# Attention scores made two query tiles at a time, with the q_high by k_low products in the two row halves of the array

## What is computed

```python
def _attn_ref(q, k, v, w1, b1, w2):          # q, k, v: (4, 8, 576, 64)
    scores = scale * np.matmul(q, k.transpose(0, 1, 3, 2))
    ...                                       # bias of each head from the relative position
    scores = scores + bias.transpose(2, 0, 1)[None, :, :, :]
    scores = scores - np.max(scores, axis=-1, keepdims=True)
    attn = np.exp(scores)
    attn = attn / (np.sum(attn, axis=-1, keepdims=True) + 1e-09)
    return np.matmul(attn, v)
def _moe_ref(x, w_in, w_out):
    h = x @ w_in
    return (h * np.cos(h)) @ w_out
def _moe2_ref(x, w_gate, w_val, w_out, rms_g):
    ...                                       # RMS norm, then silu(xn @ w_gate) * (xn @ w_val) @ w_out
```

## Time and profile before

| what | value |
|---|---|
| device time, median of 3 runs | 1208.93 us (1208.05 to 1209.38) |
| device time of the profiled execution | 1208.74 us |
| its span, first to last instruction | 1207.0 us |
| mean granted clock of the tensor engine | 0.996 of full speed |
| PE busy over the span | 97% |
| DVE, ACT, POOL busy over the span | 58%, 41%, 41% |
| first and last score matmul | 68.0 us and 325.2 us |

### The profile page before, as it was taken

One profiled execution on the slowest core, in us unless ns is written; L12 is line 12 of the kernel. 1 busy time (PEld: TensorE's weight loads), 2 busy tenths in 40 slices (PEclk: granted clock), 3 DMA queues, 4 the chain that ended last, 5 costly groups with the idle time before them and its releaser, 6 DMA issues. The chain is left out here.

```text
span 1207.0 us, 21829 instructions
## 1 busy us (share of the span) xinstructions
PE 1171.1 (97%) x7464; PEld 1078.6 (89%) x7464; DVE 704.4 (58%) x1540; ACT 496.3 (41%) x1034; POOL 490.4 (41%) x515
## 2 busy tenths in 40 slices
PE   5789999999989999999999999999999999999998
PEld 2267777777779999999999999999999999999998
DVE  8978888888889867777786887553011020210201
ACT  6967787787723433333343333111111111111111
POOL 3047777777766342525243362751111111111111
PEclk9989999999999999999999999999999999999999
DMA  5754535252144000000000011330000000000000
GB/s 172 247 174 126 170 99 170 100 188 81 56 114 123 18 2 1 0 0 0 0 0 0 0 36 35 105 114 27 1 1 26 0 26 0 0 26 0 26 0 26
DMA packets 46534, 69.06 MB, mean 57 GB/s; under 512 B 3712, under 2 KB 27424, under 8 KB 46496
## 3 DMA queue, kind: packets, MB, share of 16 engines
q1 hardware_dynamic: 46496, 68.60, 18.3%
HBM read 53.25 MB, written 15.34 MB: 57 GB/s over the span
## 5 line engine op out<-in xcount | busy, mean ns | idle before, releaser
L820 PE MATMUL banks<-x_high,w_low_rest 128*128 128x384 f32 x672 | 224.5, 334 | 0.0
L818 PE MATMUL banks<-x_high,w_high_rest 128*128 128x384 f32 x672 | 224.4, 334 | 0.0
L819 PE MATMUL banks<-x_low,w_high_rest 128*128 128x384 f32 x672 | 224.4, 334 | 0.0
L1367 DVE TENSOR_TENSOR X<-X,banks 128x384 f32<-128x384 f32 x72 | 39.8, 552 | 298.6 <-PE banks L820 298.5
L1386 POOL TENSOR_TENSOR product_low<-X,product_high 128x384 fp32r<-128x384 f32 x72 | 72.8, 1012 | 345.5 <-ACT product_high L1329 345.5
L1184 POOL TENSOR_TENSOR product_low<-g,product_high 128x384 fp32r<-128x384 f32 x96 | 102.3, 1066 | 236.9 <-ACT product_high L1066 236.9
L818 PE MATMUL bank<-product_high,w_high_rest 128*128 128x384 f32 x480 | 162.1, 338 | 0.8 <-POOL product_low L1184 0.8
L820 PE MATMUL bank<-product_high,w_low_rest 128*128 128x384 f32 x480 | 160.5, 334 | 0.0
L819 PE MATMUL bank<-product_low,w_high_rest 128*128 128x384 f32 x480 | 160.5, 334 | 0.0
L1094 ACT ACTIVATE angle<-angle,quarter 128x384 f32<-128x384 f32 x96 | 59.3, 617 | 201.9 <-DVE angle L1126 201.9
L644 DVE CUSTOM_DVE_ANT_0 probs<-banks,bias 128x576 f32<-128x576 f32 (+1 forms) x160 | 119.7, 748 | 20.6 <-PE banks L506 10.0
(11 more groups left out here) (113 smaller groups left out, 2525.4 us busy)
## 6 DMA issues: line engine op xcount, KB each, us to landing
raw_qk<-in_qk SPq DMA_DIRECT2D x32, 576.0 KB, 3.8
bias_scratch<-bias_stage SPq DMA_DIRECT2D x36, 288.0 KB, 3.2
bias<-bias_scratch SPq DMA_DIRECT2D x32, 288.0 KB, 3.4
w_raw<-in_w_out SPq DMA_DIRECT2D x28, 256.0 KB, 2.7
values<-in_v SPq DMA_DIRECT2D x16, 320.0 KB, 4.1
w_raw<-in_w_in SPq DMA_DIRECT2D x16, 256.0 KB, 2.9
out_t<-X SPq DMA_DIRECT2D x5, 768.0 KB, 3.6
w_raw<-in_w_gate SPq DMA_DIRECT2D x12, 256.0 KB, 3.3
```

The costliest lines, as they stand in the source:

```text
L818: nc.tensor.matmul(out, high, x_high, start=start, stop=False)
L819: nc.tensor.matmul(out, high, x_low, start=False, stop=False)
L820: return nc.tensor.matmul(out, low, x_high, start=False, stop=stop)
```

## The change

Tiles are scored in twos, s and s+1 with s even. Of each tile the two matmuls with `k_high` stay as they are (128 rows of the array; `both_parts`). The two with `k_low` now use the 64 partitions that hold q_high, and the other 64, q_low by k_low, are not computed any more. So that the two tiles of a two use different halves of the array, q_low lies below q_high for even tiles and above it for odd tiles. The half-row matmuls of the two tiles are issued alternately, between the full ones of tile s and those of tile s+1. PE's other work follows after both: turn(s-4), turn(s-3), then a part of mix at s = 4, 6, 8 and 0. DVE's order and the counts of `prepared` are changed to suit, and POOL subtracts q_low in three instructions for each head.

```diff
-MIX_SLOTS = (3, 5, 8, 0)
+MIX_SLOTS = (4, 6, 8, 0)
...
-            sp.wait_ge(self.prepared[h], n)
+            sp.wait_ge(self.prepared[h], n * 3)
...
     def low_part_q(self, pool, n, h):
-        pool.tensor_tensor(self.q_parts[h][D:P, 0:S], self.raw_q[h][D:P], self.q_parts[h][D:P, 0:S].bitcast(F32),
+        blocks = lambda t, rows: t[rows, 0:(NQ - 1) * P].rearrange("p (a b c) -> p a b c", b=2, c=P)
+        for odd in range(2):
+            rows = self.rows_low(odd)
+            first = (odd - h * NQ) % 2
+            high, raw = blocks(self.q_parts[h], rows)[:, :, first, :], blocks(self.raw_q[h], rows)[:, :, first, :]
+            pool.tensor_tensor(high, raw, high.bitcast(F32), ALU.subtract).then_inc(self.prepared[h], 1)
+        rows, last = self.rows_low((h * NQ + NQ - 1) % 2), slice((NQ - 1) * P, S)
+        pool.tensor_tensor(self.q_parts[h][rows, last], self.raw_q[h][rows, last], self.q_parts[h][rows, last].bitcast(F32),
                            ALU.subtract).then_inc(self.prepared[h], 1)
-        pool.wait_ge(self.prepared[h], n + 1)
+        pool.wait_ge(self.prepared[h], (n + 1) * 3)
...
+            def both_parts(n, s, start):
...
+                for half in range(2):
+                    last = nc.tensor.matmul(scores[s % 2][:, half, 0:HS], att.q_parts[h][:, qt * P:(qt + 1) * P],
+                                            att.k_high[h][:, half * HS:(half + 1) * HS], start=start, stop=not start)
+                return last
+
+            def high_by_low(n, s, half, start):
...
+                rows = att.rows_high(s % 2)
+                return nc.tensor.matmul(scores[s % 2][:, half, 0:HS], att.q_parts[h][rows, qt * P:(qt + 1) * P],
+                                        att.k_low[h][rows, half * HS:(half + 1) * HS], start=start, stop=not start)
+
+            def score_two(n, s, first):
+
+                if s == 0:
+                    pe.wait_ge(att.prepared[0], (n + 1) * 3)
+                if not (first and s == 0):
                     pe.wait_ge(biased, n * TILES + (s - 1))
+                both_parts(n, s, True)
+                if s == NQ - 1:
+                    pe.wait_ge(att.prepared[1], (n + 1) * 3)
+                if not (first and s == 0):
+                    pe.wait_ge(biased, n * TILES + s)
                 for half in range(2):
-                    for part, k_part in ((0, att.k_high[h]), (1, att.k_low[h])):
-                        last = nc.tensor.matmul(scores[s % 2][:, half, 0:HS], att.q_parts[h][:, qt * P:(qt + 1) * P],
-                                                k_part[:, half * HS:(half + 1) * HS], start=(part == 0), stop=(part == 1))
-                last.then_inc(scored, 1)
+                    done = high_by_low(n, s, half, False)
+                    high_by_low(n, s + 1, half, True)
+                done.then_inc(scored, 1)
+                both_parts(n, s + 1, False).then_inc(scored, 1)
...
             def pair(n, parity, step):
-                for s in range(TILES):
-                    slot(n, parity, s, step)
+                for s in range(0, TILES, 2):
+                    slots(n, parity, s, step)
...
+            def sum_inverse(n, parity, step, s):
+                m, _, r = back(n, parity, s, EXP_LAG)
+                if s >= EXP_LAG or step > 0:
+                    guard(m, r)
+                    invert(m, r)
...
+                for s in range(0, TILES, 2):
+                    m2, _, r2 = back(n, parity, s, EXP_LAG + 1)
                     if hp is not None:
                         dve.wait_ge(att.bias_in[s], (hp + 1) * 16)
                     add_bias(n, s, step == 0)
+                    sum_inverse(n, parity, step, s)
+                    if hp is not None:
+                        dve.wait_ge(att.bias_in[s + 1], (hp + 1) * 16)
+                    add_bias(n, s + 1, step == 0)
+                    if s >= EXP_LAG + 1 or step > 0:
+                        normalise(dve, m2, r2, dve_normed)
+                    sum_inverse(n, parity, step, s + 1)
+                    if step > 0 and s == T_LAG:
                         keep_end(n - 1, 1 - parity)
```

More of the change, by code:

```diff
@@ L354, in low_part_q, with rows_low, rows_high @@
     def low_part_q(self, pool, n, h):
-        pool.tensor_tensor(self.q_parts[h][D:P, 0:S], self.raw_q[h][D:P], self.q_parts[h][D:P, 0:S].bitcast(F32),
-                           ALU.subtract).then_inc(self.prepared[h], 1)
-        pool.wait_ge(self.prepared[h], n + 1)
+        blocks = lambda t, rows: t[rows, 0:(NQ - 1) * P].rearrange("p (a b c) -> p a b c", b=2, c=P)
[6 more added lines that the diff above has]
+        pool.tensor_tensor(self.q_parts[h][rows, last], self.raw_q[h][rows, last], self.q_parts[h][rows, last].bitcast(F32),
+                           ALU.subtract).then_inc(self.prepared[h], 1)
+        pool.wait_ge(self.prepared[h], (n + 1) * 3)
+    def rows_low(self, odd):
+        return slice(0, D) if odd else slice(D, P)
+    def rows_high(self, odd):
+        return slice(D, P) if odd else slice(0, D)
     def prepare(self, pool, n, h):
@@ L497, in _ @@
         def _(pe):
-            def score(n, s, first):
+            def both_parts(n, s, start):
                 h, qt = s // NQ, s % NQ
-                if qt == 0:
-                    pe.wait_ge(att.prepared[h], n + 1)
-                if not (first and s < 2):
-                    pe.wait_ge(biased, n * TILES + (s - 1))
+                for half in range(2):
[3 more added lines that the diff above has]
+            def high_by_low(n, s, half, start):
+                h, qt = s // NQ, s % NQ
+                rows = att.rows_high(s % 2)
[5 more added lines that the diff above has]
+                if not (first and s == 0):
+                    pe.wait_ge(biased, n * TILES + (s - 1))
+                both_parts(n, s, True)
[3 more added lines that the diff above has]
+                    pe.wait_ge(biased, n * TILES + s)
                 for half in range(2):
-                    for part, k_part in ((0, att.k_high[h]), (1, att.k_low[h])):
-                        last = nc.tensor.matmul(scores[s % 2][:, half, 0:HS], att.q_parts[h][:, qt * P:(qt + 1) * P],
-                                                k_part[:, half * HS:(half + 1) * HS], start=(part == 0), stop=(part == 1))
-                last.then_inc(scored, 1)
+                    done = high_by_low(n, s, half, False)
+                    high_by_low(n, s + 1, half, True)
+                done.then_inc(scored, 1)
+                both_parts(n, s + 1, False).then_inc(scored, 1)
             def turn(n, s, first):
@@ L553, in mix, with slots @@
                                      probs_t_end[parity][:, queries], start=False, stop=True).then_inc(mixed_ready, 1)
-            def slot(n, parity, s, step, compute=True):
+            def slots(n, parity, s, step, compute=True):
                 if compute:
[L558 to L563, removed]
+                    score_two(n, s, step == 0)
+                for r in (s, s + 1):
+                    if r < T_LAG:
+                        if step > 0:
+                            turn(n - 1, TILES - T_LAG + r, False)
+                    elif compute:
+                        turn(n, r - T_LAG, step == 0)
                 if s == MIX_SLOTS[3]:
@@ L580, in _ @@
                 pair(m * 2 + 1, 1, 2)
-            for s in range(MIX_SLOTS[1] + 1):
-                slot(PAIRS, 0, s, 2, compute=False)
+            for s in range(0, MIX_SLOTS[1] + 1, 2):
+                slots(PAIRS, 0, s, 2, compute=False)
             pe.wait_ge(biased, PAIRS * TILES)
@@ L669, in back @@
                 return (n, parity, s - by) if s >= by else (n - 1, 1 - parity, TILES + s - by)
+            def sum_inverse(n, parity, step, s):
[3 more added lines that the diff above has]
+                    invert(m, r)
             def pair(n, parity, step, hp=None):
-                for s in range(TILES):
-                    m, _, r = back(n, parity, s, EXP_LAG)
-                    m3, _, r3 = back(n, parity, s, EXP_LAG + 1)
+                for s in range(0, TILES, 2):
+                    m2, _, r2 = back(n, parity, s, EXP_LAG + 1)
                     if hp is not None:
```

## The result

The changed kernel takes 1230.73 us in the median (1229.31 to 1231.38), the kernel before 1208.49 us in the same runs: a ratio of 1.0187 (95% interval 1.0174 to 1.0199), 22 us slower. The profiled execution of the changed kernel spans 1227.5 us, 20.5 more than before.

A forecast was written before the change was run, and what follows sets the result against it. PE was taken to bound the kernel. Shape changes +0.72 net of overlap, moved steps +0.35 and a wait +0.27 made +1.34 us a pair, +20.1 over pairs 1 to 15, +1 for pair 0: 1230 us, range 1207 to 1248.

The forecast's parts named there:

- What bounds it: Attention pairs: PE sets the pace, busy 16.30 of 16.30 us; its summed steps and changes of array shape give 16.3.
- the missing 1.7 us: PE's time in a pair beyond its 14.6 us of steps, put down to changes of the array's shape in use.
- Overlap, -0.27 a group: Scores of two tiles: four half-row matmuls run as two overlapping twos, saving 0.27 us a group, 1.33 a pair.
- The first rival: Half-row score matmuls don't overlap: 1244 us if only loads are serial, 1251 if nothing overlaps; chance 0.18.
- The price of a change: Entering and leaving the half-row shape in each score group: 0.20 in, 0.21 out, +0.41 us a group.
- Moved steps, +0.35 a pair: PE's reordered turns of tiles 4 and 9: one more shape exit each, 0.14 and 0.21 us.
- The wait at tile 4: Half-row matmuls wait in mid-group for DVE's bias of s-1; stall 0.27 us a pair, in the group without mix.
- 6. *DVE.: Guard and invert stand together, some 0.35 us more a group; DVE's work becomes 16.2, still under PE's new pair.
- 7. *POOL.: Low q in three instructions instead of one: 1.8 us taken, against 1.42 before; even twice the length would be hidden.
- The sum: Per pair 0.72 + 0.35 + 0.27 = +1.34 us, +20.1 over pairs 1 to 15; whole kernel +21, to 1230.
- Pair 0 was put at +1: First pair, without mix and held by DVE: five groups with 0.2 to 0.35 us more, +1 us.

The follow-up runs named there:

- e3: The kernel before with the parts of mix at s = 4, 6, 8 and 0 instead of 3, 5, 8 and 0, nothing else; 1210.61 us.
- e2: The changed kernel with q_high in partitions 0 to 63 for every tile, so both tiles' half-row products use the same half of the array; 1249.99 us.
- e8: The kernel before with the two parts of mix of the second half of the queries made together at s = 8; 1212.67 us.
- e9: The kernel before with mix parts joined in twos, the first half's at s = 3, the second half's at s = 8; 1225.83 us.
- e1: The changed kernel with all 128 rows for the products with k_low again, order and waits as in the changed kernel; 1224.09 us.
- e7: The changed kernel with half-row products of tiles 4 to 9 after both tiles' full ones, next to mix or tile 4's turn; 1229.06 us.
- e5: The kernel before, one tile at a time, with each tile's two k_low products on only the 64 rows of q_high; 1260.44 us.

## Why the prediction was right

1230 was predicted, 1230.73 measured. By its steps:

1. *What bounds it.* PE's sum by steps, with the changes of shape as the missing 1.7 us. Confirmed by e3, where nothing but one neighbour changes and the pair grows by 0.19.
2. *Overlap, -0.27 a group.* Held: starts within 0.01 us, and +1.17 a pair in e2 without it. The first rival, with 0.18, is out.
3. *The price of a change.* I took 0.20 in (the empty stretch before the 64-row transposes and a full weight load) and 0.21 out (from mix to scores); it measured 0.19 to 0.20 each way. "All other changes between 128 and 64 show it" was too strong: my own rows had 0.14 and 0.15 where short loads followed. A group costs 0.13 net, not 0.14; a pair 0.64, not 0.72. The Trainium skill's rule ("TensorEngine Tiling (Array Packing)", Key Properties: a change of mode drains, a change of tile doesn't) fits: e2 and the changed kernel pay at the same places, e2 uses one tile and the changed kernel two.
4. *Moved steps, +0.35 a pair.* Measured 0.15 (from the 64-row transposes of tile 4 to the full ones of tile 5) + 0.19 (from those of tile 9 to the scores of tile 4, as in e3) = 0.34.
5. *The wait at tile 4.* 0.27 predicted, 0.33 measured. One term is mis-sized and another makes up for it. I put 0.133 from the first half-row product to the second of the same tile; it is 0.24, since the weights of the second two load in the open. And I put 0.11 for a load before the product that ends the wait; in the trace its recorded start is that of its load (230.20 and 230.21), and the load in the open falls behind it. Timeline of DVE in the changed kernel, for the earlier trace rows:

```profile
228.24 0.76 DVE L678 CUSTOM_DVE_ANT_0 probs<-banks,bias 128x576 f32<-128x576 f32 x1 [0.34 <-PE banks L523]
...
229.11 0.16 DVE L690 RECIPROCAL inv_total<-guarded 128x1 f32<-128x1 f32 x1
229.38 0.76 DVE L678 CUSTOM_DVE_ANT_0 probs<-banks,bias 128x576 f32<-128x576 f32 x1
230.07 0.08 DVE L678 DVE_READ_ACCUMULATOR2_ANT neg_max<- 128x1 f32 x1
230.07 0.52 DVE L426 TENSOR_SCALAR probs<-probs,inv_total 128x576 f32<-128x576 f32 x1
230.50 0.15 DVE L685 TENSOR_SCALAR guarded<-total 128x1 f32<-128x1 f32 x1
```
```profile
230.20 0.30 PEld L523 LDWEIGHTS banks<-k_low,q_parts 64*128 64x128 f32 x4 [0.49 <-DVE neg_max L678]
```

   From 227.49 to 228.24 is 0.75 instead of 0.64; 1.14 to the second add_bias, 0.77 to its end at 230.15, and 0.06 to the load at 230.21: 2.72, where 2.69 was predicted. PE's own way was 2.38 (227.49 to 229.65 and 0.22), where 2.42 was predicted, with the same two errors in it. What is left of both ways is 0.03 and 0.04.
6. *DVE.* The guard now waits for the normalise and the invert for the guard, as said. DVE did not become the bound; e8 and e9 show how near it is.
7. *POOL.* I put 1.8 for the three pieces of a head's q_low. They ran from 227.17 to 229.00, hidden: from 105 to 320 us PE waits nowhere for POOL.

```profile
227.17 1.54 POOL L362 TENSOR_TENSOR q_parts<-raw_qk,q_parts 64x256 fp32r<-64x256 f32 x2
228.68 0.32 POOL L364 TENSOR_TENSOR q_parts<-raw_qk,q_parts 64x64 fp32r<-64x64 f32 x1
```

8. *The sum.* 0.64 + 0.34 + 0.33 = 1.31 by the measured terms, 1.32 by the pairs; 1.34 was predicted. So the total rests on two errors that nearly cancel, 0.08 too much in the changes of shape and 0.06 too little in the wait. Pair 0 was put at +1 by DVE's order; it was +1.5. The first score matmul came 0.8 earlier, which nothing in the prediction has. The path, the terms and their order of size were right; that the time came out within 1 us is luck.

How does the loss divide? In the changed kernel about half of it, 0.64, is what the changes of shape cost beyond the overlap, and 0.67 is the price of the order that makes the overlap possible. Without any half rows 0.88 of the 1.32 are still lost (e1), since PE is sooner at tile 4 then and waits longer.

## What to carry to other kernels

Two half-row products in different halves of the array do run as one, but the entry into the shape and the exit cost 0.19 to 0.20 us each here, so a stretch of narrow work (products that use half of the rows or columns) must save more than 0.39 before it pays; 0.27 doesn't. Count the changes of shape in PE's order before moving anything, transposes of 64 rows included, and put narrow work of different kinds side by side. Then ask who starves: with two score buffers, the kernels that moved scores or turns further apart (e7, e8, e9) gained less than their steps of PE promised, or lost, by waits of DVE and then of PE.

## What was not expected of the hardware

The attention begins with the tensor engine at half clock in every kernel, but the length of that stretch differs. The first pair's stretches at half clock, of the kernel before, the changed one, e2 and e5 in this order (columns as in the earlier trace rows, the clock is the number after POOL):

```profile
67.70:74.50 6.80, 6.47 (x25) 5.80 (x25) 4.50 (x16) 3.17 (x7) 1.17 (x2) 0.50 0.61 182
```
```profile
66.50:76.70 10.20, 8.84 (x33) 6.46 (x34) 6.55 (x22) 4.06 (x10) 2.96 (x5) 0.50 0.72 212
```
```profile
66.10:83.20 17.10, 15.76 (x53) 12.54 (x54) 9.51 (x33) 8.09 (x19) 6.74 (x9) 0.50 0.41 129
```
```profile
68.30:92.20 23.90, 23.90 (x82) 17.93 (x81) 13.35 (x51) 12.92 (x30) 12.28 (x13) 0.50 0.33 100
```

6.8, 10.2, 17.1 and 23.9 us at 1.2 GHz before 2.4 GHz came, though PE shows no idle time in e5. The two with the most half-row work without a partner had the longest. PE's steps double there (a transpose's from 0.109 to 0.21 in e5), so this lengthens pair 0, and in e5 pair 1 too: it fits what e5 was over its expectation there. Of pair 0's +1.5 in the changed kernel it is at most a small part: e1, in the same order, had 6.8 us at half clock as before had, and its pair 0 took 14.80, 1.3 over before.

In e1, e2 and e7 a second stretch of 3.4 us at half clock follows in pair 1. Here is most of e1's:

```profile
88.90:92.20 3.30, 3.30 (x16) 2.73 (x16) 2.27 (x7) 1.43 (x6) 3.29 (x5) 0.50 0.56 181
```

PE was busy for 2.20 of the 3.3 us before it (85.5 to 88.8 us). Pair 1 took 18.62 in e1 and 19.05 in e7, against 17.24 in the changed kernel without such a stretch. So pair 1 holds 1.4 and 1.8 us of their times; the steps from pair to pair over pairs 2 to 14, on which the readings above rest, are free of it. It is one execution of each kernel, and none of the runs was made to tell what sets these stretches, so the cause stays open.
